# Turning a tile of x by DRAM and 32x32 vector blocks instead of TensorE, in a fused attention and gated MLP kernel

## The chip, the cores and the metric

The kernel runs on one core of one Trainium2 chip. The metric is device time in microseconds, from the first to the last instruction of the core; lower is better. Work is spread over TensorE (PE, with its weight loads as PEld), VectorE (DVE), ScalarE (ACT), and SyncE (SP), whose queue issues every DMA of this kernel. GpSimd (POOL) only makes constants.

## The reference: what is computed

B = 2 sequences, N = 6016 tokens, C = 256 channels, F = 1536 hidden channels, all float32.

```
qn = q / (norm(q, axis=1) + 1e-06);  kn = k / (norm(k, axis=1) + 1e-06)
s  = kn.transpose(0, 2, 1) @ qn / tau          # C x C for each sequence
a  = softmax(s, axis=-1)                       # a.sum + 1e-09 below the line
x  = (v @ a).reshape(B * N, C)
xn = x / sqrt(mean(x * x, axis=-1) + 1e-06) * rms_g
out = (silu(xn @ w_gate) * (xn @ w_val)) @ w_out
```

Attention is over channels, so q and k are read once to build one 256x256 matrix; the rest goes token by token.

## The kernel before

**Number format.** To keep float32 accuracy, an operand of the large products is held as a high part and a low part (`_hi`, `_lo`, type fp32r), and `product` (L368) makes three matmuls for each product: hi·hi, lo·hi, hi·lo. ACT writes the high part, DVE subtracts it and writes the low part.

**Prologue.** The q and k of sequence 0 are read in groups of four token blocks; TensorE accumulates their scores and ACT and DVE the squared norms. Softmax gives `a_hi`, `a_lo`. Tile 0 of x is then made (`attend`), scaled, turned by TensorE (`turn_x`, L443, called at L512) and split (`xt`, L633 and L876), so that the first `gate_val` (L515) can start. Meanwhile SP loads the pieces of the weights, which ACT and DVE split.

**Steps.** A tile is 4 blocks of 128 tokens (512 columns); there are 12 tiles in each sequence, 24 in all, and tile 11 of each has 3 blocks. One `step` works on tile t and prepares tile t+1. For f = 2 to 11 it issues `gate_val` (12 matmuls: gate and value of hidden block f, 128 channels) and `project` (6 matmuls: the hidden block f-1 into the output). Around some of these f it adds other work. On TensorE (L521 to L561):

- f = 4, in steps 0 to 7 only (`groups`): `scores1`, 24 matmuls, part of the scores of sequence 1;
- f = 5: `turn_v` (L421), 8 transposes of the tile v of t+1, which waits for v's DMA (`v_loaded`) and for the PSUM banks `ps_aux`, free when the output of tile t-1 is staged (`staged_act`, `staged_dve`);
- f = 6: `attend`, 24 matmuls, x of tile t+1 into `ps_aux`;
- f = 9: `turn_x`, 8 transposes of the scaled x (`xn`) into `ps_aux`;
- after f = 11: `gate_val` of tile t+1, block 0 (needs `xt_done`), the last `project`, `gate_val` block 1, and `turn_out`, 8 transposes of the output.

ACT and DVE follow with `unit` (silu, product, split of the hidden block) for each f, and among these: `vt` (split of v), `x_squares`, `x_rms` (12 small DVE instructions, an inverse square root), `x_scale` (ACT blocks 0 and 1, DVE blocks 2 and 3, into `xn` in SBUF), and `xt`, the split of the turned x. In steps 9 and 10 (`soft`) the softmax of sequence 1 is made too.

**SP.** The order on SP's queue is written out by hand (`step`, L311). In step t: for `groups`, wait for `acc_done`, then q and k of a coming group (L228); wait for `v_turned`, then v of tile t+1 (L233); wait for `staged_act` and `staged_dve` of tile t, then the output of tile t (L333). So the v of tile t+1 is issued just behind the output of tile t-1. Every engine runs its own program in order; semaphores join them.

Of the kernel before, what the change touches and what calls it, by code (L numbers as in the profile page):

```python
# [3 lines left out]

def attention_gated_mlp(nc, q, k, v, tau, w_gate, w_val, w_out, rms_g, out):
    f32 = mybir.dt.float32
# [6 lines left out]
    P = 128  # L33
# [18 lines left out]
    GROUP_PAIRS = (TILES - AHEAD) // 2  # L52
    NEWTON = 12
    assert H == 2 and TILES == 12 and GV_PIECES == 6 and WO_PIECES == 3 and B == 2 and AHEAD == 4

# [5 lines left out]
    val_v = w_val.rearrange("(h p) f -> p h f", p=P)  # L61
    wout_v = w_out.rearrange("(f p) c -> p f c", p=P)

    ctx = ExitStack()
    with ctx:
# [36 lines left out]
        hid_lo = sb("hid_lo", [P, 2, TC * P], f32r)  # L102
        out_t = sb("out_t", [P, H, TC * P])
        stage = sb("stage", [P, 2, GW])

# [69 lines left out]
        xn_act = sem("xn_act")  # L175
        xn_dve = sem("xn_dve")
        x_turned = sem("x_turned")
        xt_hi_done = sem("xt_hi_done")
# [25 lines left out]
        def adds(G):  # L204

            return 2 * G if isinstance(G, int) and G < TILES else 2 * G - 2

        def run_steps(eng, step):
# [31 lines left out]
        def _(sp):  # L240
# [68 lines left out]
            raw_group(sp, 1, AHEAD, TC, 0)  # L309

            def step(b, i, odd, n, nx, groups, soft):  # L311
                t = value(2 * i + odd)
                turned, staged = value(t + 1), value(t + 2)
                if groups:
                    added = value(adds(TILES + AHEAD - 1 + t))

                    sp.wait_ge(acc_done, added)
                    raw_group(sp, 1, t + 1 + AHEAD, TC, 1 - odd)
                if nx:
                    last = isinstance(t, int) and t == TILES - 1  # L320
                    if not last:

                        value(vv[b, :, bass.ds(TC * (t + 1 - TILES * b), nx), :].offset * 4)

                    sp.wait_ge(v_turned, turned)
                    if last:
                        v_tile(sp, 1, 0, nx, 0)
                    else:
                        v_tile(sp, b, t + 1 - TILES * b, nx, 1 - odd)

                sp.wait_ge(staged_act, staged)
                sp.wait_ge(staged_dve, staged)
                sp.dma_start(ov[b, :, bass.ds(TC * (t - TILES * b), n), :],  # L333
                             stage[:, odd, 0:n * C].rearrange("p (j c) -> p j c", c=C))\
                    .then_inc(slot_dma[odd], 16)
# [31 lines left out]
        def _(pe):  # L367
# [21 lines left out]
            def scores1(t, n):  # L389

                pe.wait_ge(qk_lo_done, 2 * t + 2)
                pe.wait_ge(staged_act, t + 1)
# [37 lines left out]
            def attend(x, b, n, half=False):  # L430
# [10 lines left out]
                last.then_inc(x_mm, 1)  # L441

            def turn_x(x, n):  # L443

                pe.wait_ge(xn_act, x + 1)
                pe.wait_ge(xn_dve, x + 1)
                for h in range(H):
                    for j in range(n):
                        last = nc.tensor.transpose(ps_aux[h][:, j * P:(j + 1) * P], xn[:, j, h * P:(h + 1) * P],  # L449
                                                   ident[:, :])  # L450
                last.then_inc(x_turned, 1)

# [58 lines left out]
            raw_scores(ps_out, TILES // RING + 1, 1, TC - 1, done=False)  # L511
            turn_x(0, TC)  # L512
            raw_scores(ps_out, TILES // RING + 1, 1, TC, j0=TC - 1, final=True)
# [7 lines left out]
            def step(b, i, odd, n, nx, groups, soft):  # L521
                t = 2 * i + odd
                for f in range(2, NF):
# [4 lines left out]
                    project(t, f - 1, n)  # L528
                    if groups and f == 4:
                        scores1(t, n)  # L530
                    if soft and f == 3:
                        pe.wait_ge(staged_dve, t + 1)
                        if soft == 1:
                            norms(1, ps_aux[1])
                        else:
                            spread(1, ps_aux[1])
                    if nx and f == 5:

                        if soft == 1:
                            pe.wait_ge(norms_read, 2)  # L540
                        if soft == 2:
                            pe.wait_ge(qb_copied, 2)
                        if groups:
                            pe.wait_ge(s_added, t + 2)
                        else:
                            pe.wait_ge(staged_act, t + 1)
                        pe.wait_ge(staged_dve, t + 1)
                        turn_v(t + 1, 1 - odd, i + odd + 1, nx)
                    if nx and f == 6:
                        turns = isinstance(t, int) and t == TILES - 1  # L550
                        if turns:
                            pe.wait_ge(a_done, 2)
                        attend(t + 1, b + turns, nx)
                    if nx and f == 9:
                        turn_x(t + 1, nx)
                if nx:
# [15 lines left out]
        def _(act):  # L572
# [30 lines left out]
            def attention_hi(b):  # L603
                act.wait_ge(rdiv_done, b + 1)
                for c in range(H):
                    last = nc.scalar.activation(a_hi[:, b, c, :], s_norm[:, c, :], ACT.Copy,
                                                scale=rdiv[:, c:c + 1])
# [25 lines left out]
            def xt(x, slot, n, first=False):  # L633
                act.wait_ge(x_turned, x + 1)
                for h in range(H):
                    last = nc.scalar.activation(xt_hi[:, slot, h, 0:n * P], ps_aux[h][:, 0:n * P], ACT.Copy)
                    if first and h == 0:
# [81 lines left out]
            def step(b, i, odd, n, nx, groups, soft):  # L719
                t = 2 * i + odd  # L720
                for f in range(2, NF):
                    unit(t, f, n)
                    if groups:
# [9 lines left out]
                        if f == 7:  # L733
                            squares(TILES + g, 1, odd, n, free=2 * t + 2 * TILES + 2 * AHEAD - 4)
                    if soft == 2 and f == 3:
                        copy_spread(1, ps_aux[1])
                    if soft == 2 and f == 10:
# [3 lines left out]
                    if nx:  # L741
                        if f == 5:
                            vt(t + 1, nx)
                        if f == 6:
                            x_squares(t + 1, nx)
                        if f == 8:
                            x_scale(t + 1)
                        if f == 9:
                            xt(t + 1, 1 - odd, nx)
# [15 lines left out]
        def _(dve):  # L765
# [79 lines left out]
            def attention_lo(b):  # L845
                dve.wait_ge(rdiv_done, b + 1)
                dve.wait_ge(a_hi_done, b + 1)
                for c in range(H):
                    last = nc.vector.scalar_tensor_tensor(out=a_lo[:, b, c, :], in0=s_norm[:, c, :],
                                                          scalar=rdiv[:, c:c + 1], in1=fl(a_hi[:, b, c, :]),  # L850
                                                          op0=ALU.mult, op1=ALU.subtract)
# [18 lines left out]
            def x_scale(x, n):  # L870
# [80 lines left out]
            gv_lo_piece(5, 0)  # L951
            wo_lo_piece(0, 1)
            xt(0, 0, TC, first=True)

# [12 lines left out]
            def step(b, i, odd, n, nx, groups, soft):  # L967
                t = 2 * i + odd
                for f in range(2, NF):
                    unit(t, f, n)  # L970
                    if groups:
# [3 lines left out]
                        if f == 3:  # L975
                            split_lo(t, 1, odd, n)
                        if f == 4:
                            add_scores(t)
# [4 lines left out]
                    if soft == 1 and f == 2:  # L983
                        fold_squares(1)
                    if soft == 1 and f == 3:
                        inverse_roots(1, ps_aux[1])
                    if soft == 1 and f == 6:
                        inverse_norms()
                    if soft == 2 and f == 4:
                        dve.wait_ge(s_added, TILES - AHEAD + 1)  # L990
# [3 lines left out]
                    if soft == 2 and f == 11:  # L994
                        attention_lo(1)
                    if nx:
                        if f == 5:
                            vt(t + 1, nx)
                        if f == 7:
                            x_rms(t + 1, nx)  # L1000
                        if f == 8:
                            x_scale(t + 1, nx)
                        if f == 9:
                            xt(t + 1, 1 - odd, nx)
                if nx:
# [37 lines left out]
```

## Time and profile before

| | |
|---|---|
| time, median of 3 runs | 1391.71 us (1390.07 to 1392.17) |
| the profiled execution | 1388.8 us (its span is its own time) |
| PE busy | 1372.5 us, 99% |
| PEld busy | 1169.4 us, 84% |
| DVE busy | 646.8 us, 47% |
| ACT busy | 557.7 us, 40% |
| mean granted TensorE clock | 0.998 |
| one step of a full tile without `groups` | 54.6 us |

The busy times overlap. The page follows the chain of work that ended last back from the end, and says for each group of instructions what its engine waited for. A time that stands in the chain is time of the span; an idle stretch of an engine that nobody waits for is not. The step's length is the distance of the same group of matmuls in two steps of the chain (883.07 to 937.68 us).

### The profile page before, as it was taken

The numbers are of one execution on the slowest core, as the hardware profiler recorded it, in microseconds if no ns is written. First come the engines' busy times: TensorE is split into PE (matmuls) and PEld (weight loads), VectorE is DVE, ScalarE is ACT, GpSimd is POOL, SyncE is SP. The second block draws the span as 40 slices with busy tenths as digits, with TensorE's granted clock in tenths as the row PEclk, the third lists the DMA queues.
The fourth block names the chain that finished last, engine by engine and source line by source line (L and its number), as shares of the span: only waits on it lengthen the run. The fifth ranks groups of instructions, "written<-read, shape, count | busy, mean of one in ns | idle before, by whom it ended". The sixth has DMA issues, their size and how long they took to land.

```text
span 1388.8 us, 18598 instructions
## 1 busy us (share of the span) xinstructions
PE 1372.5 (99%) x6780; PEld 1169.4 (84%) x6780; DVE 646.8 (47%) x1197; ACT 557.7 (40%) x1056; POOL 0.8 (0%) x7
## 2 busy tenths in 40 slices
PE   8999999999999999999999999999999999999998
PEld 7878888888888888888899888888888888888888
DVE  4865454454544544454444434434434344344343
ACT  5654444344443443334343333333333333333332
POOL 0000000000000000000000000000000000000000
PEclk9999999999999999999999999999999999999999
DMA  8730110101101000000000000000000000000000
GB/s 298 277 121 1 62 60 0 60 0 60 60 0 60 0 30 30 1 31 27 1 31 28 1 31 31 0 30 0 30 30 0 30 30 0 30 30 0 27 16 12
DMA packets 19335, 54.50 MB, mean 39 GB/s; under 512 B 2146, under 2 KB 7010, under 8 KB 19298
## 3 DMA queue, kind: packets, MB, share of 16 engines
q1 hardware_dynamic: 19298, 54.01, 11.2%
q8 instruction: 23, 0.38, 0.1%
q14 instruction: 14, 0.11, 0.0%
HBM read 41.68 MB, written 12.32 MB: 39 GB/s over the span
## 4 chain that ended last, share of the span: by engine, by line
PE 96%; DVE 1%; DMA 1%; ACT 1%; issue 0%; SPq 0%; DVEq 0%; ACTq 0%
PE ps_gate L373 28%; PE ps_val L373 28%; PE ps_out L373 27%; PE ps_aux L373 7%; PE ps_aux L382 2%; PE ps_aux L482 1%; PE ps_aux L426 1%; PE ps_aux L449 1%; DMA raw<-in_k_dram 1%; PE ps_out L382 0%; DVE sqr_acc L771 0%; DVE wgv_lo L913 0%; ACT sqr L577 0%; DVE hid L890 0%; ACT hid_hi L651 0%
## 5 line engine op out<-in xcount | busy, mean ns | idle before, releaser
L890 DVE TENSOR_TENSOR hid<-ps_val,sg 128x512 f32<-128x512 f32 (+1 forms) x288 | 195.8, 680 | 424.4 <-PE ps_val L373 420.5
L651 ACT ACTIVATE hid_hi<-hid 128x512 fp32r<-128x512 f32 (+1 forms) x288 | 179.5, 623 | 445.8 <-DVE hid L890 445.8
L895 DVE TENSOR_TENSOR hid_lo<-hid,hid_hi 128x512 fp32r<-128x512 f32 (+1 forms) x288 | 196.2, 681 | 201.6 <-ACT hid_hi L651 201.6
L647 ACT ACTIVATE sg<-ps_gate 128x512 f32<-128x512 f32 (+1 forms) x288 | 170.1, 591 | 249.5 <-PE ps_gate L373 248.4
L373 PE MATMUL ps_gate<-xt_hi,wgv_hi 128*128 128x512 f32 (+1 forms) x576 | 226.4, 393 | 1.7 <-DVE xt_lo L879 1.7
L373 PE MATMUL ps_out<-hid_hi,wo_hi 128*128 128x512 f32 (+1 forms) x576 | 223.8, 389 | 1.2 <-DVE hid_lo L895 1.2
L373 PE MATMUL ps_gate<-xt_lo,wgv_hi 128*128 128x512 f32 (+1 forms) x576 | 222.0, 385 | 0.0
L373 PE MATMUL ps_gate<-xt_hi,wgv_lo 128*128 128x512 f32 (+1 forms) x576 | 222.0, 385 | 0.0
L373 PE MATMUL ps_out<-hid_hi,wo_lo 128*128 128x512 f32 (+1 forms) x576 | 221.9, 385 | 0.0
L373 PE MATMUL ps_val<-xt_hi,wgv_hi 128*128 128x512 f32 (+1 forms) x576 | 221.7, 385 | 0.0
L373 PE MATMUL ps_val<-xt_hi,wgv_lo 128*128 128x512 f32 (+1 forms) x576 | 221.7, 385 | 0.0
L373 PE MATMUL ps_out<-hid_lo,wo_hi 128*128 128x512 f32 (+1 forms) x576 | 221.5, 385 | 0.0
L373 PE MATMUL ps_val<-xt_lo,wgv_hi 128*128 128x512 f32 (+1 forms) x576 | 221.4, 384 | 0.0
L373 PEld LDWEIGHTS ps_out<-hid_hi,wo_hi 128*128 128x128 f32 x576 | 108.2, 188 | 22.1 <-DVE hid_lo L895 2.3
L373 PEld LDWEIGHTS ps_gate<-xt_hi,wgv_lo 128*128 128x128 f32 x576 | 108.1, 188 | 21.2
L373 PEld LDWEIGHTS ps_val<-xt_hi,wgv_lo 128*128 128x128 f32 x576 | 108.1, 188 | 20.9
L373 PEld LDWEIGHTS ps_val<-xt_lo,wgv_hi 128*128 128x128 f32 x576 | 108.1, 188 | 20.8
L373 PEld LDWEIGHTS ps_val<-xt_hi,wgv_hi 128*128 128x128 f32 x576 | 108.1, 188 | 20.8
L373 PEld LDWEIGHTS ps_out<-hid_hi,wo_lo 128*128 128x128 f32 x576 | 108.1, 188 | 20.7
L373 PEld LDWEIGHTS ps_gate<-xt_hi,wgv_hi 128*128 128x128 f32 x576 | 108.4, 188 | 20.2 <-issue 2.1
L373 PEld LDWEIGHTS ps_out<-hid_lo,wo_hi 128*128 128x128 f32 x576 | 108.2, 188 | 19.8
L373 PEld LDWEIGHTS ps_gate<-xt_lo,wgv_hi 128*128 128x128 f32 x576 | 108.5, 188 | 18.1
(107 smaller groups left out, 1123.2 us busy)
## 6 DMA issues: line engine op xcount, KB each, us to landing
v_in<-in_v_dram SPq DMA_DIRECT2D x22, 512.0 KB, 4.2
out_dram<-stage SPq DMA_DIRECT2D x22, 512.0 KB, 2.9
raw<-in_q_dram SPq DMA_DIRECT2D x21, 512.0 KB, 4.4
raw<-in_k_dram SPq DMA_DIRECT2D x21, 512.0 KB, 5.2
stage<-in_moe_w_out_dram SPq DMA_DIRECT2D x6, 256.0 KB, 2.9
raw<-in_q_dram SPq DMA_DIRECT2D x3, 384.0 KB, 5.0
raw<-in_k_dram SPq DMA_DIRECT2D x3, 384.0 KB, 6.0
xn<-in_moe_w_gate_dram SPq DMA_DIRECT2D x3, 256.0 KB, 5.1
```

Of the source, the lines that this page charges most:

```text
L373: last = nc.tensor.matmul(ps, lhs[h][a], rhs[h][c], start=start and h == 0 and m == 0, stop=stop and h == n - 1 and m == 2)
L382: last = nc.tensor.matmul(banks[c][:, 0:C], raw[:, r, 1, j * C + c * P:j * C + (c + 1) * P], raw[:, r, 0, j * C:(j + 1) * C], start=first ...
L426: last = nc.tensor.transpose(banks[h][:, j * P:(j + 1) * P], v_in[:, slot, j * C + h * P:j * C + (h + 1) * P], ident[:, :])
L449: last = nc.tensor.transpose(ps_aux[h][:, j * P:(j + 1) * P], xn[:, j, h * P:(h + 1) * P], ident[:, :])
L482: last = nc.tensor.transpose(ps_aux[j // 2][:, at:at + P], out_t[:, c, j * P:(j + 1) * P], ident[:, :])
L647: nc.scalar.activation(sg[:, s, 0:n * P], ps_gate[s][:, 0:n * P], ACT.Silu).then_inc(silu_done, 1)
L651: nc.scalar.activation(hid_hi[:, s, 0:n * P], hid[:, s, 0:n * P], ACT.Copy)\
L890: nc.vector.tensor_tensor(hid[:, s, 0:n * P], ps_val[s][:, 0:n * P], sg[:, s, 0:n * P], ALU.mult)\
L895: nc.vector.tensor_tensor(hid_lo[:, s, 0:n * P], hid[:, s, 0:n * P], fl(hid_hi[:, s, 0:n * P]), ALU.subtract).then_inc(hid_split, 1)
```

## The change

`turn_x` leaves TensorE. SP stores the scaled tile `xn` (token on the partition) to a scratch tensor `x_rows` in DRAM, waits until it has landed (`x_stored`), and reads it back in four DMAs. The q-th fills partitions 32q to 32q+31 with channels 64q to 64q+63 of every 32nd token, in runs of 64 channels (256 bytes), into the same `xn` buffer, now seen as `x_u`. DVE then turns it in 32x32 blocks with two `transpose` instructions into `xt_f`, which is the buffer `out_t`. For this the channels of x are interleaved (`paired`, `halves` where `a_hi` and `a_lo` are written). The split `xt` reads SBUF instead of PSUM.

Since this takes longer, work inside a step moves: `turn_v` from f = 5 to 2, `attend` from 6 to 3, `x_squares` from 6 to 3, `x_rms` from 7 to 4, `x_scale` from 8 to 5, `turn_x` (now on DVE) at 9, `xt` from 9 to 10; `scores1` from 4 to 8, and the parts of the softmax of sequence 1 later too. `scores1` now waits for `xn_act`. In SP's step `pass_x` stands between v's DMA and the output's.

```
+            def pass_x(x, scaled, held, n):
+                sp.wait_ge(xn_act, scaled)
+                sp.wait_ge(xn_dve, scaled)
+                sp.dma_start(x_st[:, 0:n, :], xn[:, 0:n, :]).then_inc(x_stored, 16)
+                sp.wait_ge(x_stored, held)
+                for q in range(QUADS):
+                    sp.dma_start(x_u[q * BL:(q + 1) * BL, 0:n * C].rearrange("l (m d) -> l m d", m=n * QUADS),
+                                 x_ld[q, :, 0:n * QUADS, :]).then_inc(x_loaded, 16)
+
+            pass_x(0, 1, 16, TC)
...
+                if nx:
+                    pass_x(t + 1, scaled, held, nx)
                 sp.wait_ge(staged_act, staged)
...
-            turn_x(0, TC)
             raw_scores(ps_out, TILES // RING + 1, 1, TC, j0=TC - 1, final=True)
...
-                    if nx and f == 5:
+                    if nx and f == 2:
...
+                        pe.wait_ge(staged_act, t + 1)
                         pe.wait_ge(staged_dve, t + 1)
                         turn_v(t + 1, 1 - odd, i + odd + 1, nx)
-                    if nx and f == 6:
+                    if nx and f == 3:
...
                         attend(t + 1, b + turns, nx)
-                    if nx and f == 9:
-                        turn_x(t + 1, nx)
...
+            def turn_x(x, n):
+                dve.wait_ge(x_loaded, LOAD * (x + 1))
+                for h in range(H):
+                    last = nc.vector.transpose(
+                        xt_f[:, h, 0:n * P].rearrange("p (m l) -> p m l", l=BL),
+                        x_u[:, 0:n * C].rearrange("p (m l h) -> p h m l", h=H, l=BL)[:, h, :, :])
+                last.then_inc(x_turned, 1)
...
-                    last = nc.vector.tensor_tensor(xt_lo[:, slot, h, 0:n * P], ps_aux[h][:, 0:n * P],
+                    last = nc.vector.tensor_tensor(xt_lo[:, slot, h, 0:n * P], xt_f[:, h, 0:n * P],
```

Three places in the order of instructions. First TensorE in the second half of the loop over steps with `groups`, from the last `project` matmul before f = 3; before:

```order
L373 MATMUL ps_out<-hid_hi,wo_lo 128x512
L373 MATMUL ps_gate<-xt_hi,wgv_hi 128x512 [waits hid_done]
L373 MATMUL ps_gate<-xt_lo,wgv_hi 128x512
L373 MATMUL ps_gate<-xt_hi,wgv_lo 128x512
L373 MATMUL ps_gate<-xt_hi,wgv_hi 128x512
```

and the same place of the changed kernel (`product` is now L384):

```order
L384 MATMUL ps_out<-hid_hi,wo_lo 128x512
L434 ISA [waits staged_dve,staged_act,s_added]
L437 MATMUL ps_aux<-ident,v_in 128x128 [waits v_loaded0]
L437 MATMUL ps_aux<-ident,v_in 128x128 x7
L384 MATMUL ps_gate<-xt_hi,wgv_hi 128x512 [waits hid_done]
```

The transposes of v, with their wait for v's DMA, have come in behind the `project` of f = 2; before, three more f lay ahead of them.

Second, SP in the same loop, from the output of one step over the whole next step; before:

```order
L333 DMA out_dram<-stage 128x1024
L244 ISA
L228 ISA [waits acc_done]
L228 DMA raw<-in_q_dram 128x1024
L228 DMA raw<-in_k_dram 128x1024
L244 ISA
L233 DMA v_in<-in_v_dram 128x1024 [waits v_turned]
L333 DMA out_dram<-stage 128x1024 [waits staged_dve,staged_act]
```

and in the changed kernel:

```order
L344 DMA out_dram<-stage 128x1024
L241 ISA
L225 ISA [waits acc_done]
L225 DMA raw<-in_q_dram 128x1024
L225 DMA raw<-in_k_dram 128x1024
L241 ISA
L230 DMA v_in<-in_v_dram 128x1024 [waits v_turned]
L311 DMA x_rows<-xn 128x4x256 [waits xn_dve,xn_act]
L314 DMA xn<-x_rows 32x16x64 [waits x_stored]
L314 DMA xn<-x_rows 32x16x64 x3
L344 DMA out_dram<-stage 128x1024 [waits staged_dve,staged_act]
```

The store and the four loads of x stand behind v and ahead of the output; v keeps its place behind the output of the step before, and q and k still stand ahead of it.

Third, SP at the end of the prologue in the changed kernel; before, the rows of x_rows were not there:

```order
L262 DMA stage<-in_moe_w_out_dram 128x2x256 [waits wpiece]
L262 DMA stage<-in_moe_w_out_dram 128x2x256
L225 DMA raw<-in_q_dram 128x1024
L225 DMA raw<-in_k_dram 128x1024
L311 DMA x_rows<-xn 128x4x256 [waits xn_dve,xn_act]
L314 DMA xn<-x_rows 32x16x64 [waits x_stored]
L314 DMA xn<-x_rows 32x16x64 x3
```

The passage of tile 0 stands behind the last pieces of `w_out` and behind a group of q and k.

## Rows read from the trace of the kernel before

**Rows 1.** The page, busy time: engine, us, share, instructions.
```profile
PE 1372.5 (99%) x6780; PEld 1169.4 (84%) x6780; DVE 646.8 (47%) x1197; ACT 557.7 (40%) x1056; POOL 0.8 (0%) x7
```

**Rows 2.** The chain that ended last, by engine: share of the span.
```profile
PE 96%; DVE 1%; DMA 1%; ACT 1%; issue 0%; SPq 0%; DVEq 0%; ACTq 0%
```

**Rows 3.** Groups of instructions: transposes of x. Busy, mean ns; idle before.
```profile
L449 PE MATMUL ps_aux<-ident,xn 128*128 128x128 f32 x188 | 24.4, 272 | 1.7 <-DVE xn L872 1.7
```

**Rows 4.** Timeline of PE, step 0, around the transposes of v: start, us.
```profile
103.71 1.03 PE L426 MATMUL ps_aux<-ident,v_in 128*128 128x128 f32 x8
104.50 0.48 PE L373 MATMUL ps_gate<-xt_hi,wgv_hi 128*128 128x512 f32 x1
104.82 0.40 PE L373 MATMUL ps_gate<-xt_lo,wgv_hi 128*128 128x512 f32 x1
105.05 0.39 PE L373 MATMUL ps_gate<-xt_hi,wgv_lo 128*128 128x512 f32 x1
```

**Rows 5.** Timeline of SP's queue, start of a step with q and k.
```profile
142.89 0.37 SPq L333 DMA_DIRECT2D out_dram<-stage  x1
143.62 0.34 SPq L228 DMA_DIRECT2D raw<-in_q_dram  x1
144.06 0.51 SPq L228 DMA_DIRECT2D raw<-in_k_dram  x1
144.76 0.34 SPq L233 DMA_DIRECT2D v_in<-in_v_dram  x1
```

**Rows 6.** Timeline of PE there: first matmul of f = 2, of 3.
```profile
141.96 0.39 PE L373 MATMUL ps_gate<-xt_hi,wgv_hi 128*128 128x512 f32 x1
...
146.04 0.39 PE L373 MATMUL ps_gate<-xt_hi,wgv_hi 128*128 128x512 f32 x1
```

**Rows 7.** The tile v_in from 90 to 432 us, steps 0 to 6.
```profile
DMA to landing us min/median/max: 5.4/5.7/6.0
```

**Rows 8.** The tile v_in from 486 to 1301 us, the 16 later loads.
```profile
DMA to landing us min/median/max: 3.6/4.0/4.3
```

**Rows 9.** Timeline of SP's queue, start of a step without q and k.
```profile
917.14 0.35 SPq L333 DMA_DIRECT2D out_dram<-stage  x1
917.71 0.34 SPq L233 DMA_DIRECT2D v_in<-in_v_dram  x1
```

**Rows 10.** Timeline of PE there: first matmul of f = 2.
```profile
916.19 0.39 PE L373 MATMUL ps_gate<-xt_hi,wgv_hi 128*128 128x512 f32 x1
```

**Rows 11.** Timeline of PE, step 0: first matmul of f = 3.
```profile
88.26 0.39 PE L373 MATMUL ps_gate<-xt_hi,wgv_hi 128*128 128x512 f32 x1
```

**Rows 12.** Timeline of SP's queue, step 0: the load of v.
```profile
90.25 0.33 SPq L233 DMA_DIRECT2D v_in<-in_v_dram  x1
```

**Rows 13.** Timeline of the end of the prologue, all engines.
```profile
72.58 0.88 DVE L872 TENSOR_SCALAR xn<-ps_aux,rinv 128x256 f32<-128x256 f32 x2
...
74.71 1.08 ACT L636 ACTIVATE xt_hi<-ps_aux 128x512 fp32r<-128x512 f32 x2 [0.25 <-PE ps_aux L449]
...
75.83 1.28 DVE L879 TENSOR_TENSOR xt_lo<-ps_aux,xt_hi 128x512 fp32r<-128x512 f32 x2
...
77.26 0.47 PE L373 MATMUL ps_gate<-xt_hi,wgv_hi 128*128 128x512 f32 x1 [1.72 <-DVE xt_lo L879]
...
77.38 0.43 SPq L228 DMA_DIRECT2D raw<-in_k_dram  x1
```

**Rows 14.** The tile raw from 76 to 78 us: q and k.
```profile
DMA to landing us min/median/max: 5.2/6.0/6.7
```

**Rows 15.** The page, DMA issues: count, KB each, median us to landing.
```profile
out_dram<-stage SPq DMA_DIRECT2D x22, 512.0 KB, 2.9
```

**Rows 16.** The tile stage from 60 to 80 us: w_out, 256 KB each.
```profile
DMA to landing us min/median/max: 2.7/2.9/4.7
```

**Rows 17.** Timeline of PE, first matmul of attend in the prologue.
```profile
64.66 0.39 PE L373 MATMUL ps_aux<-a_hi,vt_hi 128*128 128x256 f32 x1 [2.43 <-DVE a_lo L849]
```

**Rows 18.** Windows there: us, busy PE, PEld, DVE, ACT, POOL, PEclk, DMA share, GB/s.
```profile
66.00:67.00 1.00, 1.00 (x7) 1.00 (x6) 1.00 (x2) 0.78 (x3) 0.00 (x0) 0.50 0.00 0
67.00:68.00 1.00, 1.00 (x6) 1.00 (x6) 1.00 (x2) 0.81 (x4) 0.00 (x0) 0.50 0.00 0
72.00:75.60 3.60, 1.93 (x12) 1.51 (x12) 3.50 (x8) 2.77 (x6) 0.00 (x0) 1.00 0.00 0
```

**Rows 19.** The chain in order of time, two stretches of attend: start, us.
```profile
64.66 4.64 PE ps_aux L373 x24
...
108.84 2.87 PE ps_aux L373 x24
```

More of the change, by code:

```diff
@@ L53, in attention_gated_mlp @@
     NEWTON = 12
+    BL = 32
+    QUADS = P // BL
+    LOAD = 16 * QUADS
     assert H == 2 and TILES == 12 and GV_PIECES == 6 and WO_PIECES == 3 and B == 2 and AHEAD == 4
@@ L62, in attention_gated_mlp @@
     wout_v = w_out.rearrange("(f p) c -> p f c", p=P)
+    x_rows = nc.dram_tensor("x_rows", [TC * P, C], f32, kind="Internal").ap()
+    x_st = x_rows.rearrange("(j p) c -> p j c", p=P)
+    x_ld = x_rows.rearrange("(m l) (i d) -> i l m d", l=BL, d=C // QUADS)
     ctx = ExitStack()
@@ L103, in attention_gated_mlp @@
         out_t = sb("out_t", [P, H, TC * P])
+        xt_f = out_t
+        x_u = xn[:, :, :].rearrange("p j c -> p (j c)")
         stage = sb("stage", [P, 2, GW])
@@ L176, in attention_gated_mlp @@
         xn_dve = sem("xn_dve")
+        x_stored = sem("x_stored")
+        x_loaded = sem("x_loaded")
         x_turned = sem("x_turned")
@@ L206, in adds, with paired, halves @@
             return 2 * G if isinstance(G, int) and G < TILES else 2 * G - 2
+        def paired(ap):
+            return ap.rearrange("p (k h) -> p h k", h=H)
+        def halves(ap):
+            return ap.rearrange("p (h k) -> p h k", h=H)
         def run_steps(eng, step):
@@ L313, in step @@
                 turned, staged = value(t + 1), value(t + 2)
+                scaled, held = value(t + 2), value(16 * (t + 2))
                 if groups:
@@ L391, in scores1 @@
                 pe.wait_ge(qk_lo_done, 2 * t + 2)
-                pe.wait_ge(staged_act, t + 1)
+                pe.wait_ge(xn_act, t + 2)
                 for c in range(H):
@@ L441, in attend @@
                 last.then_inc(x_mm, 1)
[L443 to L451, printed above, removed]
             def gate_val(tile, slot, f, n, fresh=False):
@@ L528, in step @@
                     project(t, f - 1, n)
-                    if groups and f == 4:
+                    if groups and f == 8:
                         scores1(t, n)
-                    if soft and f == 3:
-                        pe.wait_ge(staged_dve, t + 1)
+                    if soft and f == 7:
+                        pe.wait_ge(xn_dve, t + 2)
                         if soft == 1:
@@ L536, in step @@
                             spread(1, ps_aux[1])
-                    if nx and f == 5:
-                        if soft == 1:
+                    if nx and f == 2:
+                        if soft == 2:
                             pe.wait_ge(norms_read, 2)
-                        if soft == 2:
+                        if b == 0 and isinstance(t, int) and t == TILES - 1:
                             pe.wait_ge(qb_copied, 2)
[L543 to L546, printed above, removed]
+                        if groups or (b == 0 and isinstance(t, int) and t == TILES - AHEAD):
+                            pe.wait_ge(s_added, t + 1)
+                        pe.wait_ge(staged_act, t + 1)
                         pe.wait_ge(staged_dve, t + 1)
                         turn_v(t + 1, 1 - odd, i + odd + 1, nx)
-                    if nx and f == 6:
+                    if nx and f == 3:
                         turns = isinstance(t, int) and t == TILES - 1
@@ L605, in attention_hi @@
                 for c in range(H):
-                    last = nc.scalar.activation(a_hi[:, b, c, :], s_norm[:, c, :], ACT.Copy,
+                    last = nc.scalar.activation(paired(a_hi[:, b, c, :]), halves(s_norm[:, c, :]), ACT.Copy,
                                                 scale=rdiv[:, c:c + 1])
@@ L635, in xt @@
                 for h in range(H):
-                    last = nc.scalar.activation(xt_hi[:, slot, h, 0:n * P], ps_aux[h][:, 0:n * P], ACT.Copy)
+                    last = nc.scalar.activation(xt_hi[:, slot, h, 0:n * P], xt_f[:, h, 0:n * P], ACT.Copy)
                     if first and h == 0:
@@ L734, in step @@
                             squares(TILES + g, 1, odd, n, free=2 * t + 2 * TILES + 2 * AHEAD - 4)
-                    if soft == 2 and f == 3:
+                    if soft == 2 and f == 7:
                         copy_spread(1, ps_aux[1])
-                    if soft == 2 and f == 10:
+                    if soft == 2 and f == 9:
                         exponentials(1)
@@ L741, in step @@
                     if nx:
+                        if f == 2:
+                            vt(t + 1, nx)
+                        if f == 3:
+                            x_squares(t + 1, nx)
                         if f == 5:
[L743 to L746, printed above, removed]
                             x_scale(t + 1)
-                        if f == 9:
+                        if f == 10:
                             xt(t + 1, 1 - odd, nx)
@@ L848, in attention_lo @@
                 for c in range(H):
-                    last = nc.vector.scalar_tensor_tensor(out=a_lo[:, b, c, :], in0=s_norm[:, c, :],
-                                                          scalar=rdiv[:, c:c + 1], in1=fl(a_hi[:, b, c, :]),
+                    last = nc.vector.scalar_tensor_tensor(out=paired(a_lo[:, b, c, :]),
+                                                          in0=halves(s_norm[:, c, :]), scalar=rdiv[:, c:c + 1],
+                                                          in1=fl(paired(a_hi[:, b, c, :])),
                                                           op0=ALU.mult, op1=ALU.subtract)
@@ L952, in _ @@
             wo_lo_piece(0, 1)
+            turn_x(0, TC)
             xt(0, 0, TC, first=True)
@@ L976, in step @@
                             split_lo(t, 1, odd, n)
-                        if f == 4:
+                        if f == 8:
                             add_scores(t)
@@ L984, in step @@
                         fold_squares(1)
-                    if soft == 1 and f == 3:
+                    if soft == 1 and f == 7:
                         inverse_roots(1, ps_aux[1])
-                    if soft == 1 and f == 6:
+                    if soft == 1 and f == 8:
                         inverse_norms()
-                    if soft == 2 and f == 4:
+                    if soft == 2 and f == 8:
                         dve.wait_ge(s_added, TILES - AHEAD + 1)
@@ L996, in step @@
                     if nx:
+                        if f == 2:
+                            vt(t + 1, nx)
+                        if f == 4:
+                            x_rms(t + 1, nx)
                         if f == 5:
[L998 to L1001, printed above, removed]
                             x_scale(t + 1, nx)
                         if f == 9:
+                            turn_x(t + 1, nx)
+                        if f == 10:
                             xt(t + 1, 1 - odd, nx)
```

## The prediction

> **What bounds the kernel now.** I read the busy times first: PE is busy 99% of the span, DVE 47%, ACT 40% [rows 1]. The chain of waits agrees: 96% of it is PE [rows 2]. So whatever leaves TensorE's program shortens the span by what it took there, and whatever makes TensorE wait lengthens it by the whole wait; the other engines have room. TensorE takes its program in order, so next I asked at which points the changed order makes it wait for something that was long ready before. For that I put the timeline of PE beside that of SP's queue at the start of a step.
>
> **What is removed.** The profile counts 188 transposes of x with a mean of 272 ns [rows 3], but they overlap, so the mean is not the price. The timeline of an equal block, 8 transposes of v, shows it: the block starts at 103.71, the next matmul at 104.50, and that one takes 0.32 until its successor where 0.23 is usual [rows 4]. That is 0.79 + 0.09 = 0.88 us for 8. Tiles 1 to 23 hold 21 blocks of 8 and two of 6: 21 x 0.88 + 2 x 0.66 = 19.8 us gone. Tile 0 is in the prologue, below.
>
> **v's DMA is late at the new place.** Before a step with q and k, SP issues the output at 142.89, then q, k, and v at 144.76 [rows 5]. The order shows that v keeps this place. Landing takes 5.4 to 6.0, median 5.7, since q and k run ahead of it [rows 7]: it lands at 150.5. In the changed order TensorE wants v behind the `project` of f = 2, which is where f = 3 started: 146.04, that is 4.08 after f = 2 began [rows 6]. Before, v was wanted three f later, so the wait was hidden. Now it is 150.5 - 146.04 = 4.4 us, TensorE being first in line with nothing to do: everything else of the step is queued behind it. Steps 1 to 6 give 6 x 4.4 = 26.4 us. The wait cannot shorten itself by being late, as SP issues the output, and so v, at a fixed distance from the step's start.
>
> Step 0: f = 3 started at 88.26 [rows 11], v was issued at 90.25 [rows 12] because its queue waits for `acc_done`, which DVE gives after the last weight pieces. It landed about 5.5 later, 95.8: a wait of 7.5 us.
>
> Steps 7 to 22 load no q and k. v is issued at 917.71 [rows 9] and lands in 4.0 [rows 8]: 921.7. f = 2 began at 916.19 [rows 10], so TensorE is there at 920.27: 1.4 to 1.5 us. With the other half of the loop, where SP takes 0.4 more in front of v, I take 1.5 x 16 = 24 us.
>
> **The prologue.** Before, x was scaled at 73.46, turned, split into high (1.08) and low (1.28), and `gate_val` began at 77.26 [rows 13]. Now SP reaches the store only behind the pieces of w_out and the q and k issued up to 77.38 [rows 13]. This k needed up to 6.7 us [rows 14], to 84.1, and the store queues behind it. A store of this size lands in 2.9 alone [rows 15]; so it lands at 80.8 if nothing were ahead of it and at 87.0 if it started after k. I take 85.5, near the latter, since the DMA engines have 2 MB to move there. The four loads have no like in the trace. From below: 2.7, the quickest 256 KB of w_out with runs of 1 KB [rows 16]. From above: 2048 runs of 256 bytes against 256 runs, so at most 8 x 2.9 = 23. I take 5.5, near the slowest of these, 4.7, which had company in the queue. So x is back at 91.1. The two vector transposes are unseen too: no less than the 0.64 of a low split for as many elements, no more than double; I take 0.7 each. Then 1.08 + 1.28 and some 0.2 between: `gate_val` begins at 95.1, 17.8 us late. With the bounds of store and loads it is 10 to 37.
>
> The Trainium skill (DMA: Bandwidth & Descriptors, "Specifications" and "Why small descriptors are slow") asks for 512 bytes or more in a run for full rate and puts an overhead of 27% on a 256-byte one. As an estimate from that page, the loads would take v's 4.0 us [rows 8] times 1.27, 5.1 instead of my 5.5, and the sum would hardly move; no row here shows runs of 256 bytes.
>
> **The clock.** In the prologue TensorE was idle for 2.43 us before `attend` [rows 17], and soon after the granted clock was 0.50, that is 1.2 GHz, until about 68.8 [rows 18]. The 24 matmuls took 4.64 us there and 2.87 at full clock [rows 19]: 1.77 us lost. With 1.93 us busy of 3.6, idle in one piece of 1.7, the clock stayed at 1.00, 2.4 GHz [rows 18]. So I charge 1.77 to each wait above 2.43 us: the prologue and steps 0 to 6, 8 x 1.77 = 14.2 us, and nothing to the 16 short ones.
>
> **What lies beside other work.** The rest costs nothing while its cover holds. DVE gets two transposes per tile, 33 us over the kernel, at 47% busy. ACT and DVE do `vt`, squares and scaling three f earlier and the scores' sum later, in the same gaps. The scaled x of a tile is ready with f = 5, and DVE wants it back with f = 9: four times 4.08 = 16.3 us, and 2.87 more with `scores1` [rows 6, 19]. Store and loads need 2.9 + 5.5 = 8.4. `xt` ends about 1.4 us ahead of the first matmul of the next tile; beyond that cover a us late is a us lost. Splitting from SBUF instead of PSUM I leave at nothing. The output's DMA now stands behind the passage of x in SP's queue, but is wanted only at the step's end.
>
> **Sum.** -19.8 + 26.4 + 7.5 + 24 + 17.8 + 14.2 = +70.1 us; 1388.8 + 70.1 = 1458.9 for a profiled execution. The median of the runs lies 2.9 above the profile's: 1462.
>
> **Rivals.** (A) The clock stays full in the long waits. For it: one fall is all the trace has, and it came with little work around it. Against: the waits of 4.4 are longer. 1462 - 14 = 1448.
>
> (B) The short waits cost clock too. Each is 1.5 us of idle, followed by 8 transposes that take 0.8; if these were as idle, 2.3 us would come near the 2.43 of [rows 17]. Against it stands the stretch 72 to 75.6 [rows 18], idle 1.7 and then 8 transposes of x, with no fall. It would give 16 x 1.77 = 28 more: 1490. The Trainium skill (TensorE: Matmul & The Clock Gate, "Part 4: PE-mode transpose") says that transposes do not count as a busy PE. By that rule the trace should have shown a fall near 75 and does not.
>
> (C) v is in time after all, so the change is not slower. Its place is the wait for `v_loaded` at f = 2, its price the 26.4 + 7.5 + 24 and 12.4 of clock. It decides where the landing is within 2.6 us of the issue in the later steps, or v is issued a step ahead. For it: v's buffer is free a step earlier, and the waits for it showed none before. Against: SP's order still issues it behind the output, and no landing was under 3.6 [rows 8]. It gives 1388.8 - 19.8 + 17.8 + 1.8 + 2.9 = 1391.5, no change; with the prologue's store at its lower bound 1384, faster.
>
> (D) x comes back too late. The wait is then in front of the next tile's `gate_val`. The cover is about 18 us in a later step and 21 with `scores1`; with loads of 23 the passage takes 26: 16 x 8 + 7 x 5 = 163 us, and 17 more in the prologue, 1640. It begins to cost at loads of 15 us. Against: 15 us for 512 KB is three times the slowest transfer of like size here.
>
> **How the numbers follow.** Forecast 0.65, with 1448 to 1476 as its own range (the landing times and the store). A 0.12, B 0.09, C 0.04 (half no change, some of the rest faster), D 0.07, all else slower 0.03. The range reaches from below A, which with a quick prologue is at 1440, to B at 1490. A measurement of this kernel tells no change from one of about 0.2%, 2.8 us. Faster by more 0.015, within 0.025, slower 0.96.
>
> **What would show it.** Right: idle time of PE at the first transpose of v (L437), about 4.4 us in six steps, 7.5 in step 0, 1.5 in 16; released by the DMA of v. The first `gate_val` near 95. Granted clock 0.50 after the long waits alone. No idle of DVE at the vector transposes beyond the prologue. Wrong: a PE without idle at L437 (C), an idle PE at the `gate_val` of f = 0 in each step (D), or vector transposes far above 0.7 us.

## The result and the profile after

| | before | after |
|---|---|---|
| median | 1390.91 us (4 runs, 1390.07 to 1392.17) | 1464.8 us (4 runs, 1463.66 to 1468.9) |
| profiled span | 1388.8 us | 1467.1 us |

The ratio of after to before is 1.0539 (95% interval 1.0523 to 1.0555). The forecast was 1462 us, slower. The profiled execution of after is the slowest of its four, so its span grew by 78.3 us where the median grew by 73.9.

The page of the changed kernel, busy times (answers to [rows 1]) and the chain that ended last by engine ([rows 2]):

```profile
PE 1375.4 (94%) x6592; PEld 1164.2 (79%) x6592; DVE 674.2 (46%) x1245; ACT 557.1 (38%) x1056; POOL 0.8 (0%) x7
...
PE 82%; DMA 9%; DVE 3%; issue 2%; SPq 2%; ACT 1%; DVEq 0%; ACTq 0%
```

TensorE lost 188 instructions and yet is busy as long as before, since part of its work ran at half clock; and 9% of the span now passes through DMAs. Who waited for whom says which. Columns: waiting engine and line, released by, us in total, times, longest.

```profile
PE ps_aux L437 <- DMA v_in<-in_v_dram: 55.8, 23, 7.6
...
PE ps_gate L384 <- DVE xt_lo L885: 21.9, 1, 21.9
```

All 23 transposes of v after tile 0 wait for v's DMA: 55.8 us, where before there was no such row. And the first `gate_val` waits 21.9 us, where it was 1.72 [rows 13].

The queue of SP and TensorE in step 1, which answer to [rows 5, 6]: q and k and v keep their distances to the output (v 1.89 us behind it, before 1.87), and TensorE is idle for 4.26 us.

```profile
173.81 0.38 SPq L344 DMA_DIRECT2D out_dram<-stage  x1
174.55 0.37 SPq L225 DMA_DIRECT2D raw<-in_q_dram  x1
175.01 0.49 SPq L225 DMA_DIRECT2D raw<-in_k_dram  x1
175.70 0.33 SPq L230 DMA_DIRECT2D v_in<-in_v_dram  x1
```

```profile
181.41 1.97 PE L437 MATMUL ps_aux<-ident,v_in 128*128 128x128 f32 x8 [4.26 <-DMA v_in<-in_v_dram]
...
938.83 1.09 PE L437 MATMUL ps_aux<-ident,v_in 128*128 128x128 f32 x8 [1.52 <-DMA v_in<-in_v_dram]
```

The first row is step 1, the second a later step without q and k. The eight transposes take 1.97 us in the first and 1.09 in the second: behind the long wait the clock is at half. The windows of this stretch, of the same one in step 0, and around step 11 (us, busy PE, PEld, DVE, ACT, POOL, PEclk, DMA share, GB/s) answer to [rows 18]:

```profile
119.00:120.00 1.00, 1.00 (x7) 1.00 (x6) 0.00 (x0) 0.00 (x0) 0.00 (x0) 0.50 0.00 0
...
181.00:188.00 7.00, 6.59 (x21) 5.59 (x22) 1.29 (x2) 1.68 (x3) 0.00 (x0) 0.55 0.01 4
...
560.00:567.00 7.00, 7.00 (x44) 6.28 (x43) 3.56 (x5) 3.59 (x12) 0.00 (x0) 1.00 0.00 0
...
778.00:781.40 3.40, 1.21 (x11) 1.19 (x11) 0.56 (x1) 0.29 (x2) 0.00 (x0) 0.97 0.38 140
781.40:785.00 3.60, 3.60 (x14) 3.60 (x13) 1.29 (x2) 1.51 (x3) 0.00 (x0) 0.55 0.00 0
```

The granted clock fell to 0.50, 1.2 GHz, during or just behind each of the seven long waits; behind the short ones (560 to 567 is step 7, after a wait of 1.17) it stayed at 2.4 GHz, with one exception in step 11, where it fell at 781.2.

The timeline of the prologue, which answers to [rows 13]:

```profile
75.58 0.88 DVE L870 TENSOR_SCALAR xn<-ps_aux,rinv 128x256 f32<-128x256 f32 x2
...
80.92 0.38 SPq L311 DMA_DIRECT2D x_rows<-xn  x1
89.22 1.93 SPq L314 DMA_DIRECT2D xn<-x_rows  x4
...
93.71 1.31 DVE L877 STREAM_TRANSPOSE out_t<-xn 128x512 f32<-128x512 f32 x2 [14.80 <-DMA xn<-x_rows]
...
95.05 1.15 ACT L633 ACTIVATE xt_hi<-out_t 128x512 fp32r<-128x512 f32 x2 [17.60 <-DVE out_t L877]
...
96.23 1.29 DVE L885 TENSOR_TENSOR xt_lo<-out_t,xt_hi 128x512 fp32r<-128x512 f32 x2 [1.21 <-ACT xt_hi L633]
...
97.67 0.77 PE L384 MATMUL ps_gate<-xt_hi,wgv_hi 128*128 128x512 f32 x1 [21.93 <-DVE xt_lo L885]
```

The store is issued 4.5 us after x was scaled and holds the queue for 8.3 us until it has landed; the four loads are back 4.5 us after the first issue; the two vector transposes take 1.31. In a step the same passage is out of the way: the timelines of SP and DVE in step 1 show the loads issued up to 207.3 and the transposes at 220.4, not waiting.

```profile
202.43 0.38 SPq L311 DMA_DIRECT2D x_rows<-xn  x1
205.36 1.92 SPq L314 DMA_DIRECT2D xn<-x_rows  x4
```

```profile
220.41 1.30 DVE L877 STREAM_TRANSPOSE out_t<-xn 128x512 f32<-128x512 f32 x2
```

### The profile page after: what moved, and what is told of

It is laid out like the page before. It is cut to its first block, busy times and chain, and to the rows that moved or that the text cites. A ratio compares the mean times of both kernels' runs of the same rounds, so it can differ in the third digit from the quotient of the medians.

```text
span 1467.1 us, 18414 instructions
## 1 busy us (share of the span) xinstructions
PE 1375.4 (94%) x6592; PEld 1164.2 (79%) x6592; DVE 674.2 (46%) x1245; ACT 557.1 (38%) x1056; POOL 0.8 (0%) x7
## 4 chain that ended last, share of the span: by engine, by line
PE 82%; DMA 9%; DVE 3%; issue 2%; SPq 2%; ACT 1%; DVEq 0%; ACTq 0%
PE ps_gate L384 25%; PE ps_val L384 24%; PE ps_out L384 22%; DMA v_in<-in_v_dram 7%; PE ps_aux L384 6%; PE ps_aux L437 2%; PE ps_aux L393 2%; DMA raw<-in_k_dram 1%; DVE hid L896 1%; DVE stage L1022 1%; ACT hid_hi L648 1%; SPq L344 1%; SPq L225 1%; DMA x_rows<-xn 1%; PE ps_out L393 0%
## 5 line engine op out<-in xcount | busy, mean ns | idle before, releaser
L384 PE MATMUL ps_gate<-xt_hi,wgv_hi 128*128 128x512 f32 (+1 forms) x576 | 228.8, 397 | 21.9 <-DVE xt_lo L885 21.9
L384 PE MATMUL ps_gate<-xt_lo,wgv_hi 128*128 128x512 f32 (+1 forms) x576 | 225.6, 392 | 0.0
L384 PE MATMUL ps_gate<-xt_hi,wgv_lo 128*128 128x512 f32 (+1 forms) x576 | 225.0, 391 | 0.0
L384 PE MATMUL ps_out<-hid_hi,wo_hi 128*128 128x512 f32 (+1 forms) x576 | 223.9, 389 | 0.8 <-DVE hid_lo L901 0.8
L384 PE MATMUL ps_val<-xt_hi,wgv_hi 128*128 128x512 f32 (+1 forms) x576 | 223.2, 387 | 0.0
L384 PE MATMUL ps_val<-xt_lo,wgv_hi 128*128 128x512 f32 (+1 forms) x576 | 222.8, 387 | 0.0
L384 PE MATMUL ps_val<-xt_hi,wgv_lo 128*128 128x512 f32 (+1 forms) x576 | 222.7, 387 | 0.0
L384 PE MATMUL ps_out<-hid_hi,wo_lo 128*128 128x512 f32 (+1 forms) x576 | 221.7, 385 | 0.0
L384 PE MATMUL ps_out<-hid_lo,wo_hi 128*128 128x512 f32 (+1 forms) x576 | 221.5, 385 | 0.0
L384 PEld LDWEIGHTS ps_gate<-xt_hi,wgv_hi 128*128 128x128 f32 x576 | 110.7, 192 | 41.6 <-issue 22.3
L384 PEld LDWEIGHTS ps_gate<-xt_hi,wgv_lo 128*128 128x128 f32 x576 | 110.4, 192 | 22.0
L384 PEld LDWEIGHTS ps_val<-xt_hi,wgv_hi 128*128 128x128 f32 x576 | 109.6, 190 | 21.3
L384 PEld LDWEIGHTS ps_gate<-xt_lo,wgv_hi 128*128 128x128 f32 x576 | 110.8, 192 | 19.3
L384 PEld LDWEIGHTS ps_val<-xt_lo,wgv_hi 128*128 128x128 f32 x576 | 109.3, 190 | 21.2
L384 PEld LDWEIGHTS ps_val<-xt_hi,wgv_lo 128*128 128x128 f32 x576 | 109.0, 189 | 21.0
L384 PEld LDWEIGHTS ps_out<-hid_hi,wo_hi 128*128 128x128 f32 x576 | 108.2, 188 | 21.4 <-DVE hid_lo L901 1.7
L384 PEld LDWEIGHTS ps_out<-hid_hi,wo_lo 128*128 128x128 f32 x576 | 108.1, 188 | 20.8
L384 PEld LDWEIGHTS ps_out<-hid_lo,wo_hi 128*128 128x128 f32 x576 | 108.2, 188 | 19.8
```

Of the source, the lines that this page charges most:

```text
L384: last = nc.tensor.matmul(ps, lhs[h][a], rhs[h][c], start=start and h == 0 and m == 0, stop=stop and h == n - 1 and m == 2)
```

## The experiments

Seven kernels, one of them run twice. Those of one table shared the runs of before.

| run | median us | ratio to before (95%) |
|---|---|---|
| e1: v one tile ahead | 1390.5 | 0.9998 (0.9986 to 1.0011) |
| e2: tile 0 turned on TensorE | 1446.26 | 1.0387 (1.0366 to 1.0408) |
| e3: both | 1370.57 | 0.9843 (0.9818 to 0.9868) |
| e4: before, v's transposes at f = 2 | 1468.39 | 1.0548 (1.0527 to 1.0569) |

| run | median us | ratio to before (95%) |
|---|---|---|
| e5: v ahead of q and k | 1428.62 | 1.0265 (1.0248 to 1.0283) |
| e6: x's store first in the prologue | 1452.93 | 1.0446 (1.0429 to 1.0464) |
| e7: e3 and 8 more transposes a step | 1390.59 | 0.9997 (0.9987 to 1.0006) |

### e1: is it v's late issue?

```
             pass_x(0, 1, 16, TC)
+            v_tile(sp, 0, 1, TC, 1)
...
-                    sp.wait_ge(v_turned, turned)
-                    if last:
-                        v_tile(sp, 1, 0, nx, 0)
-                    else:
-                        v_tile(sp, b, t + 1 - TILES * b, nx, 1 - odd)
...
                     pass_x(t + 1, scaled, held, nx)
+                if isinstance(t, int):
+                    x = t + 2
+                    if x < ALL:
+                        sp.wait_ge(v_turned, turned)
+                        v_tile(sp, x // TILES, x % TILES, LAST if x % TILES == TILES - 1 else TC, odd)
+                else:
...
+                    sp.wait_ge(v_turned, turned)
+                    v_tile(sp, b, t + 2 - TILES * b, TC, odd)
```

> The changed kernel, but SP issues the v of tile t+2 in step t behind the passage of x, one tile ahead, into the buffer that is free since step t-1. My theory: TensorE's 23 waits for v (55.8 us in the trace of the changed kernel) go, and with them the half clock behind the seven long ones; a step with q and k grew by 5.7 us = -0.9 + 4.3 + 2.2, so the clock is 2.2 us in each, 7 x 2.2 = 15. 1464.8 - 56 - 15 = 1394 us, +-4. Rival: v is late because the DMA engines carry x too, and an earlier issue only meets other transfers: over 1420. Rival on the clock (the half clock costs nothing): 1409.

Measured 1390.5 us, 74 below the changed kernel and no different from before. No wait of TensorE for v is left, and no fall of the clock in the steps. The rival (contention) is out. SP's queue in step 1 of e1 shows the new place of v, 30 us ahead of the output of that step:

```profile
183.58 0.38 SPq L311 DMA_DIRECT2D x_rows<-xn  x1
186.50 1.93 SPq L314 DMA_DIRECT2D xn<-x_rows  x4
188.63 0.36 SPq L230 DMA_DIRECT2D v_in<-in_v_dram  x1
218.81 0.36 SPq L342 DMA_DIRECT2D out_dram<-stage  x1
```

### e2: the passage of tile 0

```
-            pass_x(0, 1, 16, TC)
...
+            def turn_x0():
...
+                        last = nc.tensor.transpose(ps_aux[h][:, j * P:(j + 1) * P],
+                                                   xn[:, j, :].rearrange("p (k h) -> p h k", h=H)[:, h, :],
+                                                   ident[:, :])
...
-            turn_x(0, TC)
             xt(0, 0, TC, first=True)
```

> The changed kernel, but tile 0 alone is turned on TensorE in the prologue, as before. My theory: the passage of tile 0 costs 17.4 us on the path and 1.8 of half clock behind it, and nothing later gives any of it back: 1464.8 - 19 = 1446 us, +-3. Rival: part of it only moves (step 0 waits for the last pieces of w_out or for the v of tile 1 by that much more): 1455 or more.

Measured 1446.26 us, 18.5 less than the changed kernel: nothing of the passage is given back later. The waits for v stay as they were:

```profile
PE ps_aux L436 <- DMA v_in<-in_v_dram: 56.8, 23, 7.7
```

### e3: both

> Both: v one tile ahead, and tile 0 turned on TensorE. My theory: only the removed transposes are left, 19.8 us less than before: 1390.9 - 19.8 = 1371 us, up to 1375 if something small stays. Rival: the passage of x has a cost in the steps that the long waits for v hide now (DVE's two transposes, x back too late): 1385 or more.

Measured 1370.57 us (the median of four), 20.5 below before. Three executions lay within 1368.7 to 1370.7; a fourth took 1694.7 us and is left out of the ratio. The mean granted clock was 0.754 in that one and 0.998 to 0.999 in the other three, so, as an estimate from the two levels 0.50 and 1.00, TensorE had half clock for about half of it. Since a version to be used must not do that, it ran again:

> The kernel with v one tile ahead and tile 0 turned on TensorE once more, in more executions, since one of the four before took 1694.7 us. My theory: its time is 1370 to 1372 us and that execution was a disturbance of its own. Rival: the version has a second, slower way to run (a wait that is sometimes missed): again an execution far above 1372.

Measured 1370.73 us (4 runs, 1370.31 to 1372.65), ratio 0.9858 (0.9841 to 0.9874). The long execution did not come back, here or in the ten executions of e7. What took the clock away in it stays open. This version beats both kernels: it is 1.4 to 1.6% below before and 6.4% below the changed kernel.

### e4: the move without the passage

```
-                    if nx and f == 5:
+                    if nx and f == 2:
...
-                        if f == 5:
+                        if f == 2:
                             vt(t + 1, nx)
```

with the waits for `ps_aux` moved so that it stays free of conflicts (scores and norms wait for `vt_done`, `attend` for `s_added`).

> The kernel before, x still turned on TensorE and no scratch tensor; only v's transposes and its split move from f = 5 to f = 2. My theory: the place alone makes the waits: 1390.9 + 56 + 15 = 1462 us, +-5, with 23 waits of TensorE for v's DMA of the same lengths. Rival: v is late only where x's traffic shares the queue: 1391 to 1400.

Measured 1468.39 us, 77 above before and 1.4 beyond the upper end of the theory: the move alone, with not a byte of x through DRAM, costs more than the whole change. The waits came as expected, 23 with 57.2 us in all; what was put too low is the rest. From its first `gate_val` to its end e4 took 79.8 us more than before (1470.0 - 78.67 against 1388.8 - 77.26), so 22.6 of it are not waits, where the theory had 15; its clock fell in eight steps. TensorE's waits in it:

```profile
PE ps_aux L426 <- DMA v_in<-in_v_dram: 57.2, 23, 7.2
```

### e5: v ahead of q and k

```
+                        v_tile(sp, b, t + 1 - TILES * b, nx, 1 - odd)
+
                 if groups:
                     added = value(adds(TILES + AHEAD - 1 + t))
...
                     raw_group(sp, 1, t + 1 + AHEAD, TC, 1 - odd)
```

> The changed kernel, but in SP's step v is issued ahead of q and k (and of the wait for acc_done), still behind the output. My theory: what makes the waits of steps 1 to 6 long (4.2 us) is q and k ahead of v, so they come down to the 1.5 us of the later steps: 6 x 2.7 = 16; step 0's wait (7.6) goes, as v need not wait for acc_done; and with no wait above 2.4 us the clock stays full in these seven steps, 15 us. 1464.8 - 16 - 8 - 15 = 1426 us, +-5. Rival (the half clock costs nothing, the waits alone count): 1441. Rival (q and k, issued just behind v, share the engines with it and keep it as late): over 1455.

Measured 1428.62 us, 36.2 below the changed kernel. SP's queue in step 1 and the row of waits:

```profile
165.76 0.38 SPq L344 DMA_DIRECT2D out_dram<-stage  x1
166.35 0.37 SPq L230 DMA_DIRECT2D v_in<-in_v_dram  x1
167.05 0.40 SPq L225 DMA_DIRECT2D raw<-in_q_dram  x1
167.55 0.42 SPq L225 DMA_DIRECT2D raw<-in_k_dram  x1
```

```profile
PE ps_aux L437 <- DMA v_in<-in_v_dram: 30.2, 22, 2.1
```

The waits shrank by 25.6 us, none is longer than 2.14, and the clock never fell in the steps. The rivals are out: the gain is more than the waits alone, and the place of v ahead of q and k counts. This run also gives the price of a wait beside its length, below.

### e6: x's store first in the prologue

```
             for n, piece in enumerate(range(5, GV_PIECES + WO_PIECES)):
+                if piece == GV_PIECES + 1:
+                    pass_x(0, 1, 16, TC)
```

> The changed kernel, but in the prologue SP issues the passage of tile 0 ahead of the last two pieces of w_out and of q and k. My theory: the store landed 8.3 us after its issue and was issued 4.5 us after x was scaled; alone it needs 2.9 and can go at once, so the first gate_val comes 9 to 10 us earlier: 1464.8 - 9.5 = 1455 us, +-3. Rival (the loads in runs of 256 bytes and the vector transposes are the cost of the prologue): within 3 us of 1464.8. Rival (w_out and q and k are then late in step 0): part is given back, 1459 or more.

Measured 1452.93 us, 11.9 below the changed kernel, at the favourable end. Its timeline of the prologue, SP and TensorE:

```profile
74.08 0.38 SPq L298 DMA_DIRECT2D x_rows<-xn  x1
77.00 1.93 SPq L301 DMA_DIRECT2D xn<-x_rows  x4
78.97 2.02 SPq L262 DMA_DIRECT2D stage<-in_moe_w_out_dram  x4
```

```profile
85.49 0.77 PE L385 MATMUL ps_gate<-xt_hi,wgv_hi 128*128 128x512 f32 x1 [12.22 <-DVE xt_lo L886]
```

The store takes 2.9 us instead of 8.3 and is issued 0.1 us after x is scaled (73.98) instead of 4.5. TensorE's wait falls from 21.93 to 12.22.

One more thing can be read in this run. Step 11 has the longest of the short waits in every kernel that waits for v. Here it was 2.21 us, with the same eight transposes behind it, and the clock stayed at 2.4 GHz:

```profile
767.03 1.06 PE L438 MATMUL ps_aux<-ident,v_in 128*128 128x128 f32 x8 [2.21 <-DMA v_in<-in_v_dram]
...
768.00:772.00 4.00, 4.00 (x27) 4.00 (x27) 2.16 (x4) 2.08 (x4) 0.00 (x0) 1.00 0.00 0
```

### e7: the price of eight transposes

```
+                    if nx and f == 9:
+                        pe.wait_ge(xn_dve, t + 2)
...
+                        for h in range(H):
+                            for j in range(nx):
+                                nc.tensor.transpose(ps_aux[1][:, j * P:(j + 1) * P], ident[:, :], ident[:, :])
```

> The kernel with v one tile ahead and tile 0 turned on TensorE, and 8 more transposes (of the identity, their result unused) on TensorE behind f = 9 of each step, where the transposes of x stood. My theory: each block of 8 costs its 0.88 us in full: 1370.6 + 19.8 = 1390 us, +-2. Rival (TensorE's weight loads or another engine bound the step, and the transposes ran in gaps): below 1380.

Measured 1390.59 us, 20.0 above e3: 180 transposes cost what was predicted for 180, in full.

```profile
L572 PE MATMUL ps_aux<-ident 128*128 128x128 f32 x180 | 23.4, 272 | 0.0
```

## Why the prediction was right

The terms of the sum can be measured one by one. The time from the first matmul of the first `gate_val` to the end ("tail") is free of what happened before it: 1311.5 us before (1388.8 - 77.26), 1369.4 after, 1292.9 in e1 (1388.2 - 95.27), 1290.8 in e3 (1368.6 - 77.76), 1327.3 in e5 (1426.3 - 99.00).

| step of the sum | predicted | measured | from |
|---|---|---|---|
| transposes of x gone, tiles 1 to 23 | -19.8 | -20.7 | tails of e3 and before |
| waits for v, steps 1 to 6, 0, 7 to 22 | +57.9 | +55.8 | row of waits |
| restart behind each wait | none | +4.4 | e5: its tail is 34.4 above e1's, its waits 30.2; 4.2 for 22 waits, 0.19 each |
| half clock in the steps | +12.4 | +16.3 | tail of after less e1's, 76.5, less 55.8 and 4.4 |
| prologue, scaled x to first `gate_val` | +17.8 | +17.4 | 97.67 - 75.58 against 77.26 - 72.58 |
| half clock behind the prologue | +1.8 | +2.1 | tails of e1 and e3 |
| the prologue ahead of x's scaling | none | +3.0 | 75.58 against 72.58 |
| sum | +70.1 | +78.3 | the spans: +78.3 |

The measured column is made of differences between spans, so its sum has to come out, and the half clock in the steps is what the other rows leave over. It can be read directly too. From the first transpose of v to the first matmul of `attend`, a full step with a short wait and full clock takes 5.03 to 5.06 us; steps 1 to 6 of the changed kernel took 7.81, 6.67, 7.69, 6.67, 7.65 and 6.68, which is 12.9 us more. Step 0 took 6.94 against 5.57 in e5, and step 11 took 5.62 against 4.06 in e6, both at full clock there. Together that is 15.9 us, near the 16.3.

The restart is mostly a matter of counting. The profile draws a matmul of 512 columns 0.39 us long while its successor starts 0.23 behind it, and counts a wait from the end of the row, so about 0.16 of the 0.19 us are time that had passed anyway and that the length of the wait leaves out.

The median's near hit, 1464.8 against 1462, is in part luck: the span was 8.2 us above its forecast. Two terms were missing (4.4 and 3.0) and the clock was put 4.2 too low, while waits, transposes and prologue together were put 3.4 too high. Between span and median I had added 2.9; here the median lies 2.3 below the profiled span, and that took 5.2 of the 8.2 back.

**The bound.** That TensorE's program is the span held both ways: 8 transposes less a step gave 20.7 us back (e3), 8 more took 20.0 (e7), and the waits came through whole (e1, e5).

**v's DMA.** The step that carried the forecast, and right in place and size: 7.6 us in step 0 (7.5 predicted), 4.26 in step 1 (4.4), 1.5 in the later ones (1.5). e4 shows that it belongs to the move and not to x's traffic. It was readable from before: the place of v in SP's queue, its landing time, and the time at which f = 3 began.

**The prologue.** Right to 0.4 us, with two small misses that nearly cancel, which is luck in so far as both were estimates between wide bounds. Counted from the end of the scaling (76.46; before 73.46): the store landed at +12.8 (predicted 85.5 - 73.46 = 12.0), the loads were back at +17.3 (17.6), as they took 4.5 us instead of 5.6, and `gate_val` began at +21.2 (21.6). e6 shows that the queue ahead of the store was over half of it.

**The clock.** Rival A (the clock stays full) is out by the windows, and that the half clock costs time is shown by e5: by the tails it gains 42.1 us, of which 25.6 are waits and 0.2 the one restart fewer; the other 16.3 are the clock (by the medians, which hold the uneven start of the prologue too, it gains 36.2). My price of 1.77 for a fall was somewhat low: 16.3 us for 8 falls is 2.0. Read one by one, they cost 1.4 to 2.8. In steps 1, 3 and 5 the clock fell about 1 us ahead of the transposes and was back 5.6 to 5.8 us behind their start: 2.6 to 2.8 each. In steps 2, 4 and 6 it fell as they began and was back after 3.4 to 3.6: 1.6 each. Rival B (the short waits cost too) came true in one of 16, step 11, where the wait was the longest of the short ones:

```profile
780.24 1.06 PE L437 MATMUL ps_aux<-ident,v_in 128*128 128x128 f32 x8 [2.19 <-DMA v_in<-in_v_dram]
```

So it was not safe to charge nothing below 2.43. But the length of the wait does not settle it either. In step 11 waits of 2.19 (the changed kernel), 2.21 (e2) and 2.23 us (e4) brought a fall, and waits of 2.21 (e6) and 2.14 (e5) brought none; no wait for v of 2.03 or less brought one in any trace. The Trainium skill (TensorE: Matmul & The Clock Gate, "Part 4: PE-mode transpose") says of a transpose that "it doesn't count as PE-busy the same way". With the 0.8 us of transposes behind the wait that would make 3.0 us in step 11 without a counted matmul, and as much in e6, which had no fall. So the length alone, counted with the transposes or without them, does not tell these cases apart; what does stays open.

**Rivals C and D.** C (v in time) is what e1 makes of the kernel, and it came out at 1390.5 against my 1391.5: the kernel with all waits gone and the prologue left. D (x back too late) did not happen: in step 1 the vector transposes began 18.0 us after the store was issued (220.41 against 202.43), and store and loads had landed after 7.4 (2.93 to the first load's issue, 1.5 to the last one's, 3.0 for it to land).

**Not forecast.** 3.0 us of the profiled span arose ahead of x's scaling. They are there already at the first matmul of `attend`, 67.66 against 64.66. The program of this stretch differs only in how `a_hi` and `a_lo` are written, and e1, e3 and e6, which write them the same way, start `attend` at 65.0 to 65.2. The trace of the changed kernel and that of e5, where x was scaled at 76.42, are the only ones with a fall of the clock at 54 us, in the middle of the prologue's matmuls; why it fell in these two is not shown. It may be part of why the profiled execution lies above the median.

## What to carry to other kernels

When a step is moved earlier on the engine that bounds the kernel, look up where each of its inputs is issued, and move that too: here the DMA of v stood behind the output of the last step, its landing was known to 0.3 us, and the move of its consumer by three blocks turned hidden time into 56 us of waits, and brought a fall of the clock with each long one. Taking work off the bounding engine pays in full (8 transposes 0.9 us) only if the path that replaces it has cover; where it has none, as for the first tile, keep the old path.

## What the runs showed of the hardware

- A fall of TensorE's clock ended 3.4 to 5.8 us after the wait did (the eight of the changed kernel) and cost 2.0 us on average. It came with all 28 waits of 4.03 us or more for v (seven in each of four kernels) and with none of 2.03 or less; between 2.14 and 2.23 us it came three times in five.
- A wait cost 0.19 us beside its length as the profile counts it (e5), of which about 0.16 is the overlap of matmuls.
- Four loads of 128 KB in runs of 256 bytes were back 4.5 us after the first issue, of which 1.93 was the issue of the four; 2.8 us is the median of one. That is less than the 5.5 that I had taken for all four.
- A vector transpose of 128x512 float32 in 32x32 blocks takes 686 ns, as long as a subtraction of that size (686). It reads every second element; no run has it with elements side by side, so what that costs is not shown. Of the split, DVE's subtraction takes as long from SBUF as from PSUM (686 against 685); ACT's copy, `xt_hi`, takes 616 against 595.

```profile
L877 DVE STREAM_TRANSPOSE out_t<-xn 128x512 f32<-128x512 f32 x44 | 28.5, 686 | 14.8 <-DMA xn<-x_rows 14.8
L885 DVE TENSOR_TENSOR xt_lo<-out_t,xt_hi 128x512 fp32r<-128x512 f32 x44 | 28.4, 686 | 5.9 <-ACT xt_hi L633 5.9
```
